# Turning gathered token rows on VectorE in 32x32 blocks, from loads by quadrant, in the expert stage of a fused attention and mixture-of-experts kernel

## The reference, cut to what matters

```python
attn_out = attention(q, k, v)        # 2 batches, 8 heads, 768 rows of 64; masked by hash buckets
x = attn_out.transpose(0, 2, 1, 3).reshape(1536, 512)

# mixture of experts: 1536 tokens, 512 wide, 8 experts, hidden width 1024
noisy = x @ w_gate + log1p(exp(x @ w_noise)) * noise
top2, top2_w = two_largest(noisy)    # and their softmax
for e in range(8):
    for k in range(2):
        mask = top2[:, k] == e
        h = np.maximum(x[mask] @ w1[e], 0.0)
        out[mask] += top2_w[mask, k, None] * (h @ w2[e])

# then a dense layer on all tokens: out @ w_in, a rational function, @ w_out (hidden width 2048)
```

## Time and profile before

| | us |
|---|---|
| median of 3 runs | 1015.65 (1014.74 to 1016.67) |
| the profiled execution | 1014.38 |
| its span, first to last instruction | 1012.8 |
| TensorE busy | 948.4, 94% of the span |
| VectorE busy | 593.4, 59% |
| ScalarE busy | 482.4, 48% |
| GpSimd busy | 402.4, 40% |

### The profile page before, as it was taken

One profiled execution on the slowest core, in us unless ns is written; L12 is line 12 of the kernel. 1 busy time (PEld: TensorE's weight loads), 2 busy tenths in 40 slices (PEclk: granted clock), 3 DMA queues, 4 the chain that ended last, 5 costly groups with the idle time before them and its releaser, 6 DMA issues.

```text
span 1012.8 us, 17972 instructions
## 1 busy us (share of the span) xinstructions
PE 948.4 (94%) x5797; PEld 815.1 (80%) x5798; DVE 593.4 (59%) x1257; ACT 482.4 (48%) x883; POOL 402.4 (40%) x344
## 2 busy tenths in 40 slices
PE   6999999999891999999999999998489999999998
PEld 4888888888771788888888888887379999999997
DVE  7888888888766222222222222222289878878775
ACT  3677777777660111111111111111177777777775
POOL 4411120111244635544662636610477654463222
PEclk9999999999995999999999999999699999999999
DMA  9752324231133856857775748733621110100000
GB/s 200 220 162 69 84 47 98 52 84 54 63 126 134 282 181 233 286 180 260 266 254 182 248 166 277 282 105 115 194 68 62 33 62 21 53 25 17 32 1 31
DMA packets 102082, 134.42 MB, mean 133 GB/s; under 512 B 55698, under 2 KB 57746, under 8 KB 101522
## 3 DMA queue, kind: packets, MB, share of 16 engines
q1 hardware_dynamic: 73778, 63.01, 20.7%
q0 software_dynamic: 19328, 54.53, 16.4%
q10 hardware_dynamic: 8928, 16.26, 4.7%
HBM read 114.12 MB, written 19.66 MB: 132 GB/s over the span
## 4 chain that ended last, share of the span: by engine, by line
PE 82%; DVE 9%; issue 3%; ACT 2%; POOL 2%; DMA 2%; SPq 0%; DVEq 0%; another core or an unknown queue 0%; ACTq 0%; POOLq 0%
PE ps_s L1049 17%; PE ps_o L1074 17%; PE ps_s L1121 13%; PE ps_t L1107 6%; PE ps_t L919 4%; PE ps_o L932 4%; PE ps_s L1107 3%; PE ps_m L1107 3%; PE ps_s L1060 3%; PE ps_s L910 3%; DVE mx L1201 2%; PE ps_s L911 2%; PE ps_m L885 1%; PE ps_m L1031 1%; PE ps_o L944 1%
## 5 line engine op out<-in xcount | busy, mean ns | idle before, releaser
L521 POOL TENSOR_TENSOR w_r<-raw,w_r 128x1024 f32 (+1 forms) x72 | 171.6, 2399 | 95.9 <-DMA raw<-in_moe_w 41.1
L1049 PE MATMUL ps_s<-w_r,xT 128*128 x744 | 179.1, 397 | 1.8 <-DVE xT L1407 1.8
L1074 PE MATMUL ps_o<-w_r,hT 128*128 x744 | 177.3, 394 | 3.0 <-DVE hT L1411 2.6
L1049 PEld LDWEIGHTS ps_s<-w_r,xT 128*128 128x128 f32 x744 | 139.0, 190 | 29.8 <-issue 2.3
L1074 PEld LDWEIGHTS ps_o<-w_r,hT 128*128 128x128 f32 x744 | 137.5, 188 | 31.0 <-issue 3.5
L1121 PE MATMUL ps_s<-w_r,g_r 128*128 128x512 f32 x576 | 145.4, 397 | 4.5 <-DVE g_r L1491 4.5
L1121 PEld LDWEIGHTS ps_s<-w_r,g_r 128*128 128x128 f32 x576 | 107.6, 190 | 25.1 <-issue 4.3
L770 ACT ACTIVATE hT<-ps_s 128x1024 fp32r<-128x1024 f32 x31 | 31.8, 1027 | 174.3 <-PE ps_s L1060 87.8
L641 POOL TENSOR_TENSOR m<-q,g_r 128x384 f32<-128x384 f32 x64 | 65.9, 1030 | 113.6 <-DVE g_r L1479 113.3
L700 ACT ACTIVATE prob<-ps_s,nb,sc 128x768 f32<-128x768 f32 x96 | 95.3, 993 | 22.5 <-DVE nb L1206 21.8
L774 ACT ACTIVATE h_sb<-ps_s 128x1024 f32<-128x1024 f32 x31 | 31.8, 1027 | 151.8 <-PE ps_s L1049 151.8
(11 more groups left out here) (242 smaller groups left out, 1584.8 us busy)
## 6 DMA issues: line engine op xcount, KB each, us to landing
w_r<-in_moe_w POOLq DMA_DIRECT2D x32, 1024.0 KB, 8.1
raw<-in_moe_w SPq DMA_DIRECT2D x56, 512.0 KB, 3.6
xg<-x_slots ACTq DMA_DIRECT2D x31, 256.0 KB, 3.1
y_slots<-y_sb ACTq DMA_DIRECT2D x31, 256.0 KB, 4.6
q_in<-in_q SPq DMA_DIRECT2D x16, 384.0 KB, 4.0
k_in<-in_k SPq DMA_DIRECT2D x16, 384.0 KB, 5.0
raw<-in_moe_w SPq DMA_DIRECT2D x16, 256.0 KB, 4.3
raw<-in_moe_w_in SPq DMA_DIRECT2D x8, 512.0 KB, 4.9
```

Source lines behind the costliest of these rows:

```text
L521: pool.tensor_tensor(of_chunk(buf, 1, n), raw[:, par, :], of_chunk(buf, 0, n).bitcast(F), ALU.subtract).then_inc(split_done, 1)
L1049: mm = pe.matmul(ps_s[0][:, o * 512:o * 512 + 512], xT[:, part, c * P:c * P + P], w_r[:, buf, wpart, col:col + 512], start=(c == 0 and par ...
L1074: mm = pe.matmul(ps_o[:, :], hT[:, part, c * P:c * P + P], w_r[:, buf, wpart, col:col + DM], start=(c == 0 and part == 0 and wpart == 0), ...
```

## The change

`turn_x` leaves TensorE. VectorE does it with one instruction for a slot, `dve.transpose` of 128x512, which turns each block of 32 rows and 32 columns in place and writes `ps_m`. Blocks alone would leave the quadrants of partitions where they were, so the rows are laid out beforehand:

- `x_sb` holds a token's 512 numbers in another order: first by the quarter (32 features) of each 128, then by the 128. Only L1225 changes, in its write pattern; the scatter still moves rows of 2 KB.
- `load_xg` issues four DMAs for a slot in place of one. Each fills one quadrant of 32 partitions with four runs of 128 numbers (512 B) from each of 32 partitions' token rows, so that block turns give the whole turn.

`xT` gets two buffers. ScalarE makes its high half (`xT_hi_out`), a slot ahead of its use; VectorE still makes the low half. `load_xg` runs three slots ahead instead of two and waits for `x_turned` first. GpSimd's wait counts four loads where it counted one. `slots` has 12 rounds instead of 13, and four slots written out behind them. In slot i the orders are now:

- TensorE: `turn_h(i-1)`, `up(i)`, `down(i-1)`.
- ScalarE: `hT_hi_out(i-1)`, `xT_hi_out(i+1)`, `relu(i)`, `load_xg(i+3)` with four issues, `store_y(i-2)`.
- VectorE: `split_h(i-1)`, `turn_x(i+1)`, `split_x(i+1)` (low half), `copy_y(i-1)`.

Ahead of slot 1, ScalarE issues the eight DMAs of loads 0 and 1, then `xT_hi_out(0)`, load 2, `xT_hi_out(1)`, `relu(0)` and load 3.

```diff
     def slots(eng, body):
-        body(1, None, 1, False, True)
-        body(2, None, 0, True, True)
-        with eng.Fori(0, (SLOTS - 5) // 2) as g:
+        body(1, 0, 1, False, True)
+        body(2, 0, 0, True, True)
+        with eng.Fori(0, (SLOTS - 7) // 2) as g:
...
-        for i in range(SLOTS - 2, SLOTS):
+        for i in range(SLOTS - 4, SLOTS):
...
             for loaded in xg_loaded:
-                pool.wait_ge(loaded, 16)
+                pool.wait_ge(loaded, 16 * Q)
...
             def load_xg(i, par):
                 row = act.value_load(slot_row[0:1, bass.ds(i, 1)], min_val=0, max_val=E * REGION - P)
-                act.dma_start(xg[:, par, :], x_slots[bass.ds(row, P), :]).then_inc(xg_loaded[par], 16)
+                if has(i, 2):
+                    act.wait_ge(x_turned, i - 1)
+                for g in range(Q):
+                    quad = slice(g * (P // Q), (g + 1) * (P // Q))
+                    act.dma_start(xg[quad, par, :].rearrange("i (a m) -> i a m", a=Q),
+                                  x_slots[bass.ds(row, P), g * P:g * P + P].rearrange("(a i) m -> i a m", a=Q)).then_inc(xg_loaded[par], 16)
+
+            def xT_hi_out(i, par):
+                act.wait_ge(x_turned, i + 1)
+                if has(i, 2):
+                    act.wait_ge(h_ready, i)
+                act.activation(xT[:, par, 0, :], ps_m[:, :], ACT.Copy).then_inc(xT_hi, 1)
...
             def pe_slot(i, half, par, y, nxt):
                 turn_h(i - 1)
-                up(i)
-                if not isinstance(i, int) or i + 1 < SLOTS:
-                    turn_x(i + 1, half, 1 - par)
+                up(i, par)
                 down(i - 1)
...
-                x_at = x_sb[:, bass.ds(n // (H // 2) * T + t, 1), bass.ds(n % (H // 2) * P, P)]
-                dve.tensor_tensor(x_at.rearrange("p a (h d) -> p (a h) d", h=2),
+                x_at = x_sb[:, bass.ds(n // (H // 2) * T + t, 1), :, bass.ds(n % (H // 2), 1), :]
+                dve.tensor_tensor(x_at.rearrange("p a (h g) b j -> p (a h) g (b j)", h=2),
...
-            def split_x(i):
-                dve.wait_ge(x_turned, i + 1)
-                dve.tensor_copy(xT[:, 0, :], ps_m[:, :]).then_inc(xT_hi, 1)
+            def turn_x(i, loads, par):
+                dve.wait_ge(xg_loaded[par], (i // 2 if isinstance(i, int) else loads) * (16 * Q) + 16 * Q)
+                if has(i, 1):
+                    dve.wait_ge(xT_ready, i)
+                dve.transpose(chunks(ps_m[:, :]), quads(xg[:, par, :])).then_inc(x_turned, 1)
+
+            def split_x(i, par):
                 dve.wait_ge(xT_hi, i + 1)
-                dve.tensor_tensor(xT[:, 1, :], ps_m[:, :], xT[:, 0, :].bitcast(F), ALU.subtract).then_inc(xT_ready, 1)
+                dve.tensor_tensor(xT[:, par, 1, :], ps_m[:, :], xT[:, par, 0, :].bitcast(F), ALU.subtract).then_inc(xT_ready, 1)
```

More of the change, by code:

```diff
@@ L32 @@
 DC, FC, FC2 = DM // P, FF // P, FF2 // P
+Q = 4
 WCOLS = DC * FF
@@ L76, in fused_kernel @@
     lg_head = at("lg_head", 138 * KB, [P, NT, H, 2 * E], F)
-    x_sb = at("x_sb", 144 * KB, [P, NT, DM], F)
+    x_sb = at("x_sb", 144 * KB, [P, NT, Q, DC, P // Q], F)
     o = 168 * KB
@@ L368, in slots, with has, quads, chunks @@
     def slots(eng, body):
-        body(1, None, 1, False, True)
-        body(2, None, 0, True, True)
-        with eng.Fori(0, (SLOTS - 5) // 2) as g:
+        body(1, 0, 1, False, True)
+        body(2, 0, 0, True, True)
+        with eng.Fori(0, (SLOTS - 7) // 2) as g:
             body(g * 2 + 3, g, 1, True, True)
             body(g * 2 + 4, g, 0, True, True)
-        for i in range(SLOTS - 2, SLOTS):
+        for i in range(SLOTS - 4, SLOTS):
             body(i, (i - 3) // 2, i % 2, True, False)
+    def has(i, less):
+        return not isinstance(i, int) or i >= less
+    def quads(z):
+        return z.rearrange("p (a c j) -> p c a j", a=Q, j=P // Q)
+    def chunks(z):
+        return z.rearrange("p (c a j) -> p c a j", a=Q, j=P // Q)
     def blocks(eng, body):
@@ L784, in _ @@
             load_xg(1, 1)
+            xT_hi_out(0, 0)
+            load_xg(2, 0)
+            xT_hi_out(1, 1)
             relu(0)
-            load_xg(2, 0)
+            load_xg(3, 1)
             def act_slot(i, half, par, y, nxt):
                 hT_hi_out(i - 1)
+                if not isinstance(i, int) or 1 < i + 1 < SLOTS:
+                    xT_hi_out(i + 1, 1 - par)
                 relu(i)
-                if not (isinstance(i, int) and i + 2 >= SLOTS):
-                    load_xg(i + 2, par)
+                if not isinstance(i, int) or i + 3 < SLOTS:
+                    load_xg(i + 3, 1 - par)
                 if y:
@@ L1023, in _, with up @@
             pe.wait_ge(tables_ready, 1)
[L1025 to L1032, removed]
             def expert_of(i):
                 return pe.value_load(slot_e[0:1, bass.ds(i, 1)], min_val=0, max_val=E - 1)
-            def up(i):
+            def up(i, par):
                 e = expert_of(i)
@@ L1048, in up @@
                             col = c * FF + o * 512
-                            mm = pe.matmul(ps_s[0][:, o * 512:o * 512 + 512], xT[:, part, c * P:c * P + P],
+                            mm = pe.matmul(ps_s[0][:, o * 512:o * 512 + 512], xT[:, par, part, c * P:c * P + P],
                                            w_r[:, buf, wpart, col:col + 512],
@@ L1417, in copy_y @@
                 dve.tensor_copy(y_sb[:, par, :], ps_o[:, :]).then_inc(y_ready, 1)
-            split_x(0)
-            split_x(1)
+            for i in range(2):
+                turn_x(i, 0, i)
+                split_x(i, i)
             def dve_slot(i, half, par, y, nxt):
@@ L1424, in dve_slot @@
                 if not isinstance(i, int) or i + 1 < SLOTS:
-                    split_x(i + 1)
+                    turn_x(i + 1, half + 2, 1 - par)
+                    split_x(i + 1, 1 - par)
                 copy_y(i - 1, (i - 1) // 2, 1 - par)
```

21 lines of the change are left out of this document (10 added, 11 removed).

## The result

| | before | changed |
|---|---|---|
| median, us | 1016.16 (1014.74 to 1016.86) | 1002.1 (1001.45 to 1004.66) |
| the profiled execution | 1014.38 | 1002.7 |
| its span | 1012.8 | 1001.1 |

The account below looks back on a forecast made before the run. TensorE, never idle in the expert slots, was taken as the bound. Terms: 13.4 (turns) + 1.2 (slot 1) - 0.7 (start) = 13.9 us off the median of 1015.65, giving 1001.7 us; range 998.0 to 1006.5.

Parts of the forecast that it names:

- The four turns, 0.48 us a slot: Slots 2 to 29: without TensorE's turns of x each saves 0.48 us, read from slot 30 against 29; 13.4 us.
- The closed boundary: Rival, between up and down: the slot saves the full 0.59 us, giving 998.6 us; chance 0.13.
- the smaller gain: Rival, in the slots: only 0.36 us a slot comes back, giving 1005.0 us; chance 0.07.
- Slot 1, 1.2 us: Slot 1: without the turn that waited for its load and delayed down(0), 1.2 us saved.
- The start, -0.7 us: Start of the expert stage: four issues, block turn and rounding put up(0) at 326.8 us, 0.7 us later.
- Dear issues: Rival, start of the stage: an issue takes 0.80 us, up(0) comes 3.6 us late, 1004.7 us; chance 0.06.
- No cost inside the slots: In the slots: added VectorE and ScalarE work fits their slack; the block turn may take 6.5 us before delaying anyone.
- ScalarE's queue: Rival, between relu and hT's rounding: over 1.6 us an issue uses up 7.7 us; at 2.0, 1047 us; chance 0.02.
- Load packets: Slot loads: 128 packets of 2 KB become 512 of 512 B, from some 12 to at most 17 us engine time.
- x_sb: Attention's write in runs of 32: no change from 0.29 us; rival, dearer by 14 us, 1015.7 us, chance 0.03.
- a sign of being wrong: Before the expert stage: the prediction would be wrong if the stage before 320 us were longer.
- The dry queue: Rival, between up and down: the expert read leaves TensorE's queue empty, boundary 1.07 us a slot, 1029.6 us; chance 0.05.

Follow-up runs that it names:

- turns_back: The changed kernel with four unused 128x128 turns of a constant put back on TensorE between up and down of every slot but the last: 1013.68 us, 1.0003 of the kernel before.
- the second profile: The changed kernel, unaltered, profiled again beside two further versions on the same chip: median 998.11 us, 0.9852 of the kernel before; profiled execution 997.5 us.
- loads_only: The kernel before with each slot's load issued as four DMAs by quadrant, the turn staying on TensorE: 1018.43 us, 1.0053 of the kernel before.
- round_on_act: The kernel before with the high half of xT made by ScalarE after the relu instead of by VectorE: 1013.18 us, 0.9996 of the kernel before.
- warm: The changed kernel with products of ident by ident on TensorE where it would only wait: 995.75 us, 0.9828 of the kernel before.
- read_early: The changed kernel with the expert number for down(i-1) read ahead of turn_h(i-1), not between up and down: 998.24 us, 0.9852 of the kernel before.
- the later comparison: The unaltered changed kernel measured again, on a chip where the kernel before takes 1013.12 us: 998.11 us, ratio 0.9852.
- turn_x11: The changed kernel with the block turn of slots 2 to 30 done eleven times in a row: 1063.71 us in one execution.
- warm_split: The kernel warm with SyncE issuing quadrants 2 and 3 of loads 0 and 1 while ScalarE issues 0 and 1: 995.24 us, 0.9821 of the kernel before.

## Why the prediction was right, point by point

- **The four turns, 0.48 us a slot.** Slot 30 as the model for all slots was the right row to read: 0.46 a slot came (12.25 to 11.79), 12.94 us in place of 13.4. The turns as such are worth 0.49 (`turns_back`); the 0.04 by which that kernel's slot (12.276) lies above the one of before (12.237) isn't the read, the loads or ScalarE's rounding, each of which was tried; whether it is the rest of the change, or that these turns work on another operand and bank, no run shows. The closed boundary (0.59) and the smaller gain (0.36) are both refuted. By the 81 ns of the Trainium skill (TensorE: Matmul & The Clock Gate, "Back-to-back issue gap") it would have been 0.32 a slot; the measured saving is over 1.4 times that.
- **Slot 1, 1.2 us.** 1.06 came (12.99 to 11.93). The load that `turn_x(2)` had waited for wasn't late any more. Of the missing 0.15 us 0.10 lie between the first load of `turn_h(0)` and that of `up(1)` (1.04 us before, 1.14 now).
- **The start, -0.7 us.** Two errors nearly cancelled. Issues come 0.49 us apart when the register address is set between them, not 0.39, so the fourth went out at 1.5 us, not 1.2; the rows landed 3.6 us after the first issue in place of the 3.8 forecast. `up(0)` came 0.48 later. I had ScalarE free 0.7 us before the turn's end; it was free at the same moment, and 0.3 too late in the second profile. The block turn took 0.717 where I took 0.7, the rounding 0.598 where I took 0.6. Dear issues are refuted by 328 ns. The 0.25 us that `up(0)` then took longer are within the spread of 7.01 to 8.09 us of its loads, so whether the clock's rise gives back some of a late start stays open.
- **No cost inside the slots.** Held: the room of the block turn was 6.1 us (6.5 forecast), and ScalarE's queue has room for 7.13 - 0.33 = 6.8 us of issues in a slot, where the prediction had 4 x 1.6 = 6.4.
- **Load packets.** The prediction's 12 to 17 us of engine time for a load don't come out of the packets that it names: 128 x 0.085 = 10.9 us, 512 x 0.027 = 13.8. Measured on q10, over the span: 8928 packets and 4.7% of 16 engines before, 22320 and 5.6% now, which is 432 packets and some 4.4 us more for a load. That was hidden as forecast.
- **`x_sb`.** 290 ns as before. That the stage before 320 us is longer was named as a sign of being wrong, and in the profile it began 0.98 us later. But it isn't this write: of the eleven other kernels profiled ten began between 317.2 and 317.8 us, `loads_only` and `round_on_act` with the old write and eight with the new one (`warm` began at 318.42).
- **The dry queue** is refuted: TensorE is busy for the whole of a slot, and `read_early` changes nothing.
- **What was missed.** The last `down`, +1.6 us, and the first products with `g_r`, -1.4, both by the clock; with +0.5 ahead of the latter and -0.1 for the rest, what lies behind the last `down` comes to -1.0. What was forecast came to 0.48 + 0.25 - 1.06 - 12.94 = -13.3 us where -13.9 was expected; the +1.6, the -1.0 and the stage's late start (+0.98) make -11.7 of it in the profiled spans, while the medians lie 14.1 us apart, and 15.0 in the later comparison (1013.12, 998.11). That the median fits the forecast to 0.4 us is partly chance.

## What to carry to other kernels

Where one engine is never idle, look for a place where the schedule already has the form that the change will give it, and read the gain there: it contains the boundary effects that a sum of durations misses. Before pieces are added to a load, look at the place where the load was nearly late already: here the same four-piece load cost 5 us with the old lead, and beside one load nothing that shows in the time with a slot more of it. And a wait of TensorE costs twice when the clock falls behind it; here filling a wait paid where it was filled up to the product that follows, and part of the gain was lost where a later wait grew.

## What the runs showed of the hardware

- A block turn of 128x512 float32 from SBUF to PSUM takes 717 ns on VectorE, hardly more than a copy of that size (0.69 us).
- The same wait of 2.81 us ahead of the last `down` was followed by the full clock in three kernels (5.29 to 5.32 us: the one before, `turns_back`, `round_on_act`) and by the lower one in eight (6.70 to 6.94 us). No run shows what decides it; both kernels with work in that wait had the full clock (5.30 us). The Trainium skill (TensorE: Matmul & The Clock Gate, "What's actually happening") says that the chip looks at TensorE in a rhythm that doesn't depend on the kernel. That would fit a difference that follows the moment and not the code, but no run here shows it.
- Longer waits sort more cleanly. Ahead of the first products with `g_r` in the dense layer, TensorE waited 3.14 to 3.67 us in four executions, and nine loads took 1.89 to 1.92 us; it waited 4.08 to 5.79 us in nine, and they took 3.21 to 3.49. In the slots of `turn_x11`, with some 2.1 us of waiting in each, the clock stayed at 1.00 (484 to 492 us). These are single executions of thirteen kernels, and only the edits of `warm` and `warm_split` touch what TensorE does shortly before this place.
- Products of `ident` by `ident` raised the clock from its lower to its upper level (`warm_split`, 316 to 318 us).
- A load in four pieces of 512-byte runs had landed 10.9 us after its first issue, 9.4 after its last, beside the weight traffic at the start (`loads_only`), where one of 2 KB rows took 6.9.
- Raising the block turn's count by five, or the loads' DMAs by three, changed the mean slot by no more than 0.001 us: with TensorE never idle, the loop's time stands still to that accuracy.
